# Two MLPs side by side on TensorE: half of an up step moved between the down step's halves, and y's rest summed on GpSimd instead of VectorE

## What is computed

```python
x_unf = x_pad[:, idx, :].reshape(B, S, K, H, group)   # 2 x 4096 tokens of 192, 7 taps
x = np.einsum('hk,bskhg->bshg', w, x_unf)             # w: softmax of weight over its taps
h = x @ w_in                                          # 192 -> 2048
g = np.where(h >= 1, h, np.where(h <= -1, 0.0, (h + 1) ** 2 / 4))
y = g @ w_out                                         # 2048 -> 192
h2 = y @ w_in2                                        # 192 -> 2048
out = (h2 * (1.0 / (1.0 + np.exp(-1.702 * h2)))) @ w_out2
```

## Time and profile before

| | |
|---|---|
| three runs | 1157.64, 1157.99, 1158.66 us; median 1157.99 |
| the profiled execution | 1157.41 us, of which the span from first to last instruction is 1155.7 us |
| granted TensorE clock | 0.999 of full speed (2.4 GHz) over the span |
| busy share: PE, DVE, ACT, POOL | 98%, 71%, 61%, 39% |

### The profile page before, as it was taken

How to read it: one execution, slowest core, us unless ns; L and a number is a source line. 1 busy time by engine, 2 the same in 40 slices (tenths; PEclk the granted TensorE clock), 3 DMA queues, 4 the chain that set the end, 5 groups by cost and what they waited for, 6 DMA issues and landing times.

```text
span 1155.7 us, 25576 instructions
## 1 busy us (share of the span) xinstructions
PE 1137.7 (98%) x9382; PEld 1022.4 (88%) x9382; DVE 821.7 (71%) x1191; ACT 699.5 (61%) x1213; POOL 447.1 (39%) x440
## 2 busy tenths in 40 slices
PE   7999999999999999999999999999999999999998
PEld 4767899999989999899999998889999999989987
DVE  6877777777777777776777777777777777766633
ACT  4866566566666566565566666565665565655554
POOL 5997754170723608054170622608044180000000
PEclk9999999999999999999999999999999999999999
DMA  6312102020020200102020020200102010000000
GB/s 196 96 40 76 41 14 57 3 52 12 11 54 1 56 8 15 49 4 58 3 51 12 10 54 2 56 8 15 49 3 58 4 17 14 10 6 1 15 7 23
DMA packets 108790, 36.43 MB, mean 32 GB/s; under 512 B 101012, under 2 KB 105490, under 8 KB 108688
## 3 DMA queue, kind: packets, MB, share of 16 engines
q1 hardware_dynamic: 108688, 34.93, 12.8%
HBM read 23.09 MB, written 6.29 MB: 25 GB/s over the span
## 4 chain that ended last, share of the span: by engine, by line
PE 90%; POOL 5%; DVE 2%; SPq 1%; ACT 1%; issue 1%; DMA 0%; POOLq 0%; DVEq 0%; ACTq 0%
PE acc_all L794 4%; PE acc_all L799 4%; PE h_all L732 4%; PE acc_all L805 4%; PE acc_all L802 4%; PE acc_all L797 4%; PE h_all L735 4%; PE h_all L737 4%; PE h_all L739 4%; PE acc_all L778 4%; PE acc_all L776 4%; PE h_all L741 4%; PE acc_all L782 4%; PE h_all L722 4%; PE h_all L719 4%; PE h_all L717 4%
## 5 line engine op out<-in xcount | busy, mean ns | idle before, releaser
L984 ACT ACTIVATE g_hi<-h_all 128x512 fp32r<-128x512 f32 x256 | 153.1, 598 | 203.1 <-PE h_all L743 177.4
L1144 DVE TENSOR_TENSOR g_lo<-h_all,g_hi 128x512 fp32r<-128x512 f32 x256 | 176.7, 690 | 121.8 <-ACT h_all L987 120.7
L1138 DVE TENSOR_TENSOR g_lo<-gate,g_hi 128x512 fp32r<-128x512 f32 x232 | 182.8, 788 | 110.7 <-ACT g_hi L976 104.7
L976 ACT ACTIVATE g_hi<-gate 128x512 fp32r<-128x512 f32 x232 | 146.5, 631 | 169.9 <-DVE gate L1132 168.2
L1123 DVE TENSOR_SCALAR clip<-h_all 128x512 f32<-128x512 f32 x256 | 175.8, 687 | 51.3 <-PE h_all L741 47.4
L529 POOL TENSOR_TENSOR x_conv<-x_in,tap_w 128x384 f32<-128x384 f32 (+1 forms) x29 | 30.6, 1075 | 458.6 <-DVE x_rest_a L1191 238.2
L536 POOL TENSOR_TENSOR x_conv<-x_conv,prod 128x384 f32<-128x384 f32 (+1 forms) x174 | 203.7, 1191 | 1.6
L970 ACT ACTIVATE clip<-clip,half 128x512 f32<-128x512 f32 x256 | 182.9, 715 | 16.6 <-DVE clip L1123 15.7
L1132 DVE TENSOR_TENSOR gate<-h_all,clip 128x512 f32<-128x512 f32 x232 | 160.4, 691 | 12.8 <-ACT clip L970 6.9
L987 ACT ACTIVATE h_all<-h_all 128x512 f32<-128x512 f32 x256 | 151.8, 593 | 0.0
L529 POOL TENSOR_TENSOR prod<-x_in,tap_w 128x384 f32<-128x384 f32 (+1 forms) x174 | 150.3, 887 | 3.2
(11 more groups left out here) (281 smaller groups left out, 4758.0 us busy)
## 6 DMA issues: line engine op xcount, KB each, us to landing
x_in<-in_x SPq DMA_DIRECT2D x14, 960.0 KB, 4.8
out_y<-raw SPq DMA_DIRECT2D x360, 16.0 KB, 1.4
raw<-x_conv SPq DMA_DIRECT2D x336, 16.0 KB, 1.8
raw<-in_moe_w_out SPq DMA_DIRECT2D x6, 384.0 KB, 3.6
raw<-in_moe_w_in SPq DMA_DIRECT2D x4, 512.0 KB, 3.5
raw<-in_moe_w_in SPq DMA_DIRECT2D x8, 256.0 KB, 4.5
stage<-in_moe_w_out SPq DMA_DIRECT2D x2, 384.0 KB, 7.3
x_in<-in_x SPq DMA_DIRECT2D x1, 768.0 KB, 9.2
```

The lines of the kernel that those rows point to most:

```text
L976: nc.scalar.activation(g1_hi[step.s % G_RING][:, :], gate1_of(step)[:, :], ACT.Copy).then_inc(g1_hi_ready, 1)
L984: nc.scalar.activation(g2_hi[step.s % G_RING][:, :], src, ACT.Gelu_apprx_sigmoid).then_inc(g2_hi_ready, 1)
L1138: nc.vector.tensor_tensor(g1_lo[k][:, :], gate1_of(step)[:, :], g1_hi[k][:, :].bitcast(FP32), ALU.subtract).then_inc(g1_lo_ready, 1)
L1144: nc.vector.tensor_tensor(g2_lo[k][:, :], bank2(step)[:, :], g2_hi[k][:, :].bitcast(FP32), ALU.subtract).then_inc(g2_lo_ready, 1)
```

## The change

On TensorE `begin_up` is cut in two: its first 4 matmuls stay ahead of the down step, and the other 4 (`go_on_up`) come between the down step's first 10 (`begin_down`) and its second 10 (`end_down`). The number of matmuls is the same. For y of tiles 2 to 15 ScalarE copies the rest accumulator whole (128 partitions) to y_part, in s = 0; then in s = 1 it copies the upper half down to y_shift, GpSimd adds the two in SBUF (`sum_y`), and ScalarE rounds in s = 2 instead of 1. VectorE's addition L1158 is gone, and L785's wait is for the ScalarE copy. VectorE's L1162 goes from slot s = 3 to 4, and the two transposes of x from slots 4 and 5 to 5 and 6. The tiles 0 and 1 keep VectorE's addition.

```diff
-        EARLY = dict(turn={4: [0], 5: [1]}, hi={5: [0], 6: [1]}, lo={7: [0], 8: [1]})
+        EARLY = dict(turn={5: [0], 6: [1]}, hi={5: [0], 6: [1]}, lo={7: [0], 8: [1]})
...
+        def sums_on_pool(tile):
+            return not isinstance(tile, int) or tile >= 2
...
+            def sum_y(tile):                                    # GpSimd
+                pool.wait_ge(y_shifted, tile - 1)
+                y_rest = y_part[0:DR, :]
+                nc.gpsimd.tensor_tensor(y_rest, y_rest, y_shift, ALU.add).then_inc(y_summed, 1)
+                pool.wait_ge(y_summed, tile + 1)
...
             def prepare(tile):
+                if sums_on_pool(tile - 1):
+                    sum_y(tile - 1)
...
-                    pe.wait_ge(y_from_dve, one.tile * 3 - 1)    # ahead of rest1 (L785)
+                    if sums_on_pool(one.tile - 1):
+                        pe.wait_ge(y_from_act, one.tile * 3 - 1)
+                    else:
+                        pe.wait_ge(y_summed, one.tile)
...
-                    down_both(back(tile, side, s, LAG), back(tile, side, s, BEHIND + LAG))
+                    begin_down(back(tile, side, s, LAG), back(tile, side, s, BEHIND + LAG))
+                go_on_up(back(tile, side, s, 0), back(tile, side, s, BEHIND))
+                if n is None or n >= BEHIND + LAG:
+                    end_down(back(tile, side, s, LAG), back(tile, side, s, BEHIND + LAG))
...
+                elif part == 1 and sums_on_pool(tile):          # ScalarE
+                    nc.scalar.activation(y_part[:, :], rest_acc[:, :], ACT.Copy).then_inc(y_from_act, 1)
...
+            def shift_y_rest(tile):
+                act.wait_ge(y_from_act, tile * 3 + 2)
+                nc.scalar.activation(y_shift, y_part[DR:P, :], ACT.Copy).then_inc(y_shifted, 1)
```

More of the change, by code:

```diff
@@ L186, in conv_mlp_mlp @@
         y_from_dve = sem("y_from_dve")
+        y_shifted = sem("y_shifted")
+        y_summed = sem("y_summed")
         out_copied = sem("out_copied")
@@ L636, in _ @@
             for tile in range(TILES - 4, TILES - 1):
+                sum_y(tile + 1)
                 sum_out(tile)
@@ L687, in up2 @@
                 if step.s == 0:
-                    pe.wait_ge(y_from_dve, (step.tile + 1) * 3)
+                    pe.wait_ge(y_from_dve, (step.tile + 1) * 2)
                 pe.wait_ge(g2_lo_ready, step.n - 1)
@@ L709, in begin_up @@
                 if two.s == 0:
-                    pe.wait_ge(y_from_dve, (two.tile + 1) * 3)
+                    pe.wait_ge(y_from_dve, (two.tile + 1) * 2)
                 if isinstance(two.n, int) and two.n < 2:
@@ L717, in begin_up, with go_on_up @@
                 nc.tensor.matmul(bank_2, in_hi[1][UPPER, cols2], y_lo[UPPER, :], start=False, stop=False)
+            def go_on_up(one, two):
+                cols1, cols2 = slice(one.s * P, (one.s + 1) * P), slice(two.s * P, (two.s + 1) * P)
+                x_hi, _, x_rest = x_set[one.side]
+                y_hi, _, y_rest = y_set[two.side]
+                bank_1, bank_2 = bank1(one)[:, :], bank2(two)[:, :]
                 nc.tensor.matmul(bank_1, in_lo[0][LOWER, cols1], x_hi[LOWER, :], start=False, stop=False)
@@ L762, in down_both @@
                 if first1:
-                    pe.wait_ge(y_from_dve, one.tile * 3 - 2)
+                    pe.wait_ge(y_from_dve, one.tile * 2 - 1)
                 nc.tensor.matmul(main1, w1_main[LOWER, :], hi1[LOWER, :], start=first1, stop=False)
@@ L790, in down_both, with end_down @@
                 nc.tensor.matmul(rest2, w2_rest[UPPER, :], lo2[UPPER, :], start=False, stop=False).then_inc(rest2_half, 1)
+            def end_down(one, two):
+                last1, last2 = one.s == F_TILES - 1, two.s == F_TILES - 1
+                w1, w2 = w_down[0][:, one.s, :], w_down[1][:, two.s, :]
+                hi1, lo1 = g1_hi[one.s % G_RING], g1_lo[one.s % G_RING]
+                hi2, lo2 = g2_hi[two.s % G_RING], g2_lo[two.s % G_RING]
+                w1_main, w1_rest, w1_lo = w1[:, 0:DM], w1[:, DM:DM + 2 * DR], w1[:, D + DR:2 * D]
+                w2_main, w2_rest, w2_lo = w2[:, 0:DM], w2[:, DM:DM + 2 * DR], w2[:, D + DR:2 * D]
+                main1, rest1 = (t[:, :] for t in acc1)
+                main2, rest2 = (t[:, :] for t in acc2)
                 pe.wait_ge(main_half, one.n - (BEHIND - 1))
@@ L818, in down1 @@
                 if first and later:
-                    pe.wait_ge(y_from_dve, step.tile * 3 - 2)
+                    pe.wait_ge(y_from_dve, step.tile * 2 - 1)
                 nc.tensor.matmul(main[:, :], w_main, hi[:, :], start=first, stop=False)
@@ L822, in down1 @@
                 if first and later:
-                    pe.wait_ge(y_from_dve, step.tile * 3 - 1)
+                    pe.wait_ge(y_summed, step.tile)
                 nc.tensor.matmul(rest[:, :], w_rest, hi[:, :], start=first, stop=False)
@@ L1080, in slot @@
                     take_y(tile - 1, 1 - side, 1)
-                if takes_y(tile) and at_y == 1:
+                if takes_y(tile) and at_y == 1 and sums_on_pool(tile - 1):
+                    shift_y_rest(tile - 1)
+                if takes_y(tile) and at_y == (2 if sums_on_pool(tile - 1) else 1):
                     take_y(tile - 1, 1 - side, 2)
@@ L1220, in slot @@
                 at_y = s - shift_y(tile)
-                if takes_y(tile) and not solo and at_y == 3:
+                if takes_y(tile) and not solo and at_y == (4 if sums_on_pool(tile - 1) else 3):
                     take_y(tile - 1, 1 - side, 2)
@@ L1233, in slot @@
                     residue1(before1)
-                if takes_y(tile) and not solo and s == 1:
+                if takes_y(tile) and not solo and s == 1 and not sums_on_pool(tile - 1):
                     take_y(tile - 1, 1 - side, 1)
```

10 lines of the change are left out of this document (5 added, 5 removed).

## The result

The changed kernel takes 1161.18 us (median of 22 runs, 1160.56 to 1162.12), the kernel before 1157.82 on the same chips (22 runs). The ratio is 1.0027, with an interval of 1.0020 to 1.0033. The predicted 1158.1 is 3.1 us low. The time lies inside the range, near its upper end, but the most likely case, "within 0.2%", did not come: this is slower by just over 0.2%. The profiled execution took 1160.75 us, its span is 1159.0.

What follows compares the result with a forecast made beforehand. The prediction took TensorE, busy 1137.7 of 1155.7 us, as the bound. Terms -5.0 + 3.6 + 0.7 + 0.4 + 0.45 = +0.15 us gave 1157.6 profiled, 1158.1 us as median, range 1154.2 to 1161.6.

Steps and rivals of the forecast that it cites:

- within 0.2%: Whole kernel: the forecast itself, net change within 0.2% of the time before; chance 0.59.
- The half wait goes: Second down half no longer waits for main_half in ordinary slots: 4.307 instead of 4.333, 193 x 0.026 = -5.0 us.
- s = 10: +3.6 us forecast: Output slots of tiles 2 to 15: L780's load 0.37 late for g1_lo, costing 0.26 in each of 14.
- lateness less 0.11: Rule for TensorE's weight loads: a late load costs its lateness less 0.11 us.
- Rival B: g1_lo not late at s = 10 and s = 2, or absorbed better: mostly around 1155 us; chance 0.20.
- s = 2: +0.7 and +0.4 forecast: y slots: L780 late for g1_lo, L785's wait gone; +0.08 in nine tiles, +0.10 in four over the back edge.
- Tile 2 and the start-up: Tile 2 loses +0.45 us at VectorE's y sum; start-up slots 26 to 33 cost 0, upper bound 1 us.
- No cost for y's sum: ScalarE's extra copy and GpSimd's 1.29 us addition fit in idle time; ScalarE's wait is covered three times.
- rival C: GpSimd's y addition holds up L1138 in s = 2, costing some 0.7 in 13 tiles: +9, 1167 us; chance 0.04.
- Rival D: New order makes its own recovery pattern in ordinary slots: +5 us or more; chance 0.06.

## Why the prediction was right in its mechanism and 3 us low

**The half wait goes: -5.0 us.** Right. Ordinary slots are 4.307 instead of 4.333, as they are in every kernel with the new order and in none without it. That they get no shorter with two pairs than with one shows that the wait lacked 0.02 and no more.

**s = 10: +3.6 us forecast, 14 slots of 0.26.** Right in place, too small. In tiles 3 to 13 the slots are 4.63 to 4.73 long, and over tiles 3 to 15 the sum is +4.1 where 13 x 0.26 = 3.4 stood. Two inputs of the step were off in tile 9: L1185 took 0.83 instead of the 0.78 of the earlier trace rows, because GpSimd's L537 runs 0.28 into it where L529 ran 0.23, and the copy L1050 began some 0.03 later than the row gave. Together the load is 0.08 later. The rule "lateness less 0.11" itself holds: the prediction keeps the recovery of 0.026 in these slots, so the price stands on 4.333, and 0.45 - 0.11 = 0.34 gives 4.67; it measures 4.68. In tiles 14 and 15, where GpSimd has no convolution left, the slots are 4.53 and 4.56. Rival B, g1_lo not late or absorbed better, is refuted by this and by the slots with the old order.

**s = 2: +0.7 and +0.4 forecast.** In tile 9 L787 (L764 of before) stood 0.25 for VectorE's y_lo, then the load of L803 stood 0.23 for L1185 and came 0.36 after its due time (2.044 after L841), where 0.32 was forecast:

```profile
613.47 0.39 PE L841 MATMUL acc_all<-g_lo,w_down 64*128 64x512 f32 x1
613.90 0.60 ACT L1033 ACTIVATE y_hi_a<-acc_all 128x512 fp32r<-128x512 f32 x1 [1.42 <-PE acc_all L840]
...
614.91 0.59 ACT L1035 ACTIVATE y_part<-acc_all 128x512 f32<-128x512 f32 x1
615.14 0.68 DVE L1185 TENSOR_TENSOR g_lo<-gate,g_hi 128x512 fp32r<-128x512 f32 x1
...
615.27 0.18 PEld L787 LDWEIGHTS acc_all<-g_hi,w_down 64*128 64x128 f32 x1 [0.25 <-DVE y_lo_a L1201]
...
615.87 0.18 PEld L803 LDWEIGHTS acc_all<-g_lo,w_down 64*128 64x128 f32 x1 [0.23 <-DVE g_lo L1185]
...
618.66 0.63 ACT L1044 ACTIVATE raw<-y_part 64x512 f32<-64x512 f32 x1
...
619.37 1.29 POOL L552 TENSOR_TENSOR y_part<-y_part,raw 64x512 f32<-64x512 f32 x1 [14.95 <-ACT raw L1044]
```

The slots are 4.57 instead of 4.54, which is 4.333 and 0.36 less 0.11. The copy with 128 partitions takes 0.59, no longer than the one with 64, and ends at 615.50, before g1_lo does: the last wait is g1_lo's, as the step said. The four tiles over the back edge were priced with their own, earlier; but that row had its head start from a stall one or two slots earlier (s = 0 took 4.44 to 4.47 there), and this stall is gone in the new order (4.31). So these four cost 0.21 each in s = 2, and give 0.12 back in s = 0 beyond the ordinary 0.026. Together s = 2 cost +1.9 and the back edge gave -0.5: 1.4 net, 1.1 forecast.

**Tile 2 and the start-up: +0.35 and "0, with 1 us as the upper bound".** Tile 2 is the step that failed by most: +1.4. I took it that a g1_lo set by VectorE's own queue keeps its time and that the room around it remains. Up to slot 31 the sum came out at 0 by luck: slots 27 to 31 took 1.0 more (L1185 took 2.87 in slot 27 where the earlier trace rows has 1.91), and slot 26 happened to end 1.0 earlier, as it ends anywhere from 91.2 to 99.4 in these kernels. In tile 2 the room is gone. On the timeline of slot 46 (tile 2, s = 14):

```profile
177.73 2.44 POOL L544 TENSOR_TENSOR x_conv<-x_conv,prod 128x384 f32<-128x384 f32 x2
177.82 1.48 DVE L1235 TENSOR_TENSOR x_lo_b<-raw,x_hi_b 128x512 fp32r<-128x512 f32 x1
...
179.22 1.50 DVE L1185 TENSOR_TENSOR g_lo<-gate,g_hi 128x512 fp32r<-128x512 f32 x1
...
180.77 0.18 PEld L803 LDWEIGHTS acc_all<-g_lo,w_down 64*128 64x128 f32 x1 [0.67 <-DVE g_lo L1185]
```

GpSimd's convolution (L544) runs under both, and both take over twice their 0.7. Before, in this slot:

```profile
177.01 0.72 DVE L1188 TENSOR_TENSOR x_lo_b<-raw,x_hi_b 128x512 fp32r<-128x512 f32 x1
...
177.15 1.46 POOL L536 TENSOR_TENSOR x_conv<-x_conv,prod 128x384 f32<-128x384 f32 x1
...
177.79 1.36 DVE L1138 TENSOR_TENSOR g_lo<-gate,g_hi 128x512 fp32r<-128x512 f32 x1
...
179.85 0.18 PEld L780 LDWEIGHTS acc_all<-g_lo,w_down 64*128 64x128 f32 x1
```

There only one of the two was stretched, and L780's load had 0.65 of room (free at 179.20, came at 179.85). The 0.45 of earlier arrival would have left 0.20; now that both are stretched, L803 is late and the slot 0.51 longer. The Trainium skill, SBUF — State Buffer, section "Who interferes with whom", has VectorE and GpSimd share a port pair that only one holds at a time; the traces agree, and give the size. L536 ends at 178.61, 0.82 after L1138's start, and L1138 takes 1.36; in s = 10 L537 ends 0.28 after L1185's start, and L1185 takes 0.83: each time what was left of GpSimd's instruction, and 0.55 more. Over the ten traces 666 g1_lo of this form start while a GpSimd tensor_tensor is running (with over 0.15 of it left), and 665 of them take what is left of it plus 0.54 to 0.56. The gate, one of whose inputs is an h bank, takes 0.70 at most beside one (805 times). So a g1_lo of 1.9 or 1.5 is not set by VectorE's own queue, as the step had it, but by the place of GpSimd's instruction under it.

That place moves from kernel to kernel, and the order doesn't settle it alone: the slot is 4.85 in the changed kernel and with the order alone, and 4.31 with the old order at s = 2 and 10, where s = 14 has the new one. In s = 2 of tile 2, where only VectorE's sum was priced (+0.45), three loads stand in the changed kernel: L787 0.28 for g1_hi, L803 0.39 for a g1_lo that took 0.96, L811 0.41 for the sum; the slot is 5.19 for 4.45. It is 4.72 with the old order at s = 2 and 10, and, with the old order in the whole tile, 5.19 in one kernel and 4.45 in the other (one pair). With y alone it is 5.36, in a profiled execution that began some 7 us late. So it is not always the order's doing. What puts GpSimd's instructions where they are in each kernel was not settled.

**No cost for y's sum.** Right for the slots: ScalarE never waits for it, and rival C, L552 ahead of g1_lo, shows nowhere: L552 starts at 619.37, and the L1185 of its slot (s = 3) is over 0.01 before; so it is in tiles 3 to 15. Wrong for the end: the part behind slot 255 is 67.0 to 67.2 in the six kernels with GpSimd's sum and 66.4 to 66.6 in the four without. Some 0.4 of it lies behind the last matmul, in the wait for the last stores (4.55 to 4.60 from its start to the end with GpSimd's sum, 4.15 or 4.16 without), though the last store is issued at the same distance. So it goes with the y edit; how stays open.

**One late slot** (s = 6 of tile 14, 4.65) was not in the sum, +0.3. It is there in the kernels with one pair and with the old order at s = 2 and 10 (4.61, 4.62), smaller where both are joined (4.39), and at s = 7 with VectorE's sum (4.81, 4.63), but not in the kernel before, and hardly with y alone (4.36). In the changed kernel ScalarE begins g2_hi (L1023) at 977.35, 1.2 later than in its rhythm, after an idle stretch of 2.34 in which it waited for nothing that the profile shows; g1_hi and g1_lo follow late, and L787 stands 0.18, L803 0.36. In the kernel before ScalarE begins g1_hi (L976) 0.65 late in the same slot, and the room takes it. So the new order lays open a pause of ScalarE; where the pause comes from stays open.

**Rival D** (a recovery pattern of the new order's own) is refuted by 4.307.

**Slots s = 15** were taken as ordinary and keep 0.25 in all. There L1185 takes 1.52 to 1.55 in tiles 3 to 13 (0.75 to 1.12 before), since GpSimd's L544 starts just ahead of it, and it ends as L803's load falls due: in tile 9 the load is 0.045 late.

In short: the terms -5.0, s = 10 and s = 2 were right in sign and place, and the 3.1 us are +1.1 in tile 2, +0.7 in s = 10, +0.6 at the end, +0.3 in s = 2, +0.3 in one slot and some +0.2 in s = 15. That they did not come to more is in part the luck of the start-up.

## What to carry to other kernels

A stall of 0.02 us a slot was worth 5 us, and one pair of matmuls in front of the wait was enough to remove it: ask how much a wait lacks, and move no more than that. Work that is moved ahead meets its inputs earlier; list the slots in which the input is anchored to something that does not move (here the end of the down step, through ScalarE's copy), and leave the old order there: 1152.3 instead of 1161.2. And room measured in one slot is not room in all: where a VectorE instruction with two inputs in SBUF starts under a running GpSimd one, it took up to twice its time and more, and an edit elsewhere can shift which slots those are.

## What the runs showed of the hardware

- A weight load only 0.015 us late cost 0.026 in each of some 200 slots; later loads cost their lateness less 0.11 on top of that: 0.36 late made a slot of 4.57 and 0.45 late one of 4.68, where 4.307 is undisturbed. This held to 0.01 there, and to 0.03 for the half wait made later (0.23 late, 4.487).
- From the start of a matmul that raises a semaphore to the load that waits for it: 0.44, at both distances tried. From VectorE's end to the load: 0.05.
- The loop's back edge cost 0.11 to 0.13 in slot s = 0 with the old order (4.44 to 4.47; 4.40 to 4.51 with the y edit), and nothing with the new one (4.31; 4.33 once, with one pair). With the half wait made later, which keeps the old order, it cost 0.01 at most (4.493 for 4.487), so it isn't the place of `begin_up` alone. Why was not looked for.
- VectorE's g1_lo took 0.68 to 0.70 alone, and 0.83, 1.50 or 2.87 where it started under a running GpSimd tensor_tensor: what was left of that instruction, plus 0.55 (665 of 666 times in ten traces).
